# Fused local attention, spatial-gating layer and gated convolution layer on one NeuronCore: shorter input rings, an earlier split of the spatial weights and a new order of the LayerNorm steps

## The chip, the cores and the metric

The kernel runs on one core of a Trainium2 chip. The metric is the device time of one execution in microseconds (us); smaller is better.

## The reference

Three layers, one after the other, all in float32:

```python
# 1. attention, batch 2 x 8 heads, 768 positions, head size 64, in chunks of 32 queries
k_full = concat([mem_k, k[16 before the chunk : 8 after it]])     # 8 memory keys + window
a = softmax(scale * q_c @ k_full.T);  out_c = a @ v_full
# 2. spatial gating
h = gelu_tanh(x @ w_in);  u, v = h[..., :512], h[..., 512:]
v_n = (v - mean(v)) / sqrt(var(v) + 1e-6) * g_ln
v_s = einsum('ts,bsd->btd', w_sg, v_n) + b_sg
y = x + (u * v_s) @ w_out
# 3. gated convolution
h = relu(y @ w_in2);  c = 3-tap convolution of h along the sequence
result = (h * sigmoid(c)) @ w_out2
```

## The kernel before

Every engine has its own instruction list, written out in Python in the order in which it runs, and the lists are tied together by semaphores. An engine never overtakes a waiting instruction of its own.

**Products.** Each product of layers 2 and 3 is made with both operands as a high part in fp32r plus a low part (the rest), so a tile is hi·hi + hi·lo + lo·hi (`product`, L403 to L413). Weights come by DMA as 256 KB chunks into a ring of two places, `raw`. A chunk j is split by `split_hi` (L334, one copy, on ACT, POOL or DVE) and `split_lo` (L352, a subtraction, on POOL for the chunks told of here). Chunks 0 to 3 are `wv`, 4 to 7 `wu`, 8 to 16 the spatial weights `sg`, 17 on are the later layers. Chunk j may be loaded only when the low part of chunk j-2 is made (`load_chunk`, L377).

**Attention** works on 16 pairs n (two heads, half the sequence). For each pair: PE `scores(n)` (mask product and q·k); DVE `take_max`; ACT `set_bias`, eight `exps`, `guard_sum`; DVE `invert_sum`; POOL `normalise_rows` (L956, two multiplications); PE `transposes`; DVE `copy_transposed`; PE `attend`; DVE `x_parts` (L605, a cast and a subtraction that make x hi and lo); ACT `copy_x` (L768). PE runs 18 passes i (L498 to L509): in pass i it does scores of pair i, transposes of pair i-2 and attend of pair i-2 (up to pass 4 of pair i-3; pass 5 attends 2 and 3). q/k and v of a pair lie in rings of four places each; SP loads them and the chunks in one in-order list that `load_order` sorts by hand-given times (L118).

**F tiles.** From pass 6 on, PE has up to two tiles of x @ w_in in each pass (`F_SLOTS`, L73): f0 to f27, seven for each quarter of the sequence (three v tiles of 128 x 512 and four u tiles of 128 x 384; in the last quarter the u tiles f21 to f24 come first and the v tiles f25 to f27 last). The first 21 F tiles and the attend outputs share two PSUM banks in turn (`RING`), so a tile waits until the entry two before it has been evicted: f18 waits for the eviction of f17, f19 for that of f18, f20 for that of f19, f0 for `copy_x(2)`, f1 for `copy_x(3)`. ACT evicts (`evict`, L774).

**LayerNorm** has twelve v tiles i. Each goes through ACT `gelu_v(i)` (into `vw`, a ring of three 2 KB places), DVE `statistics(i)`, POOL `invert_std(i)` (an addition and a power on 128x1), DVE `normalise(i)` (L630), ACT `vn_hi_part(i)` (L803), POOL `vn_lo_part(i)` (L964). For tiles 9 to 11 the eviction is the gelu itself.

**Order around the end of attention.** Chunks 13 to 16 (`C_LATE` = 13 on) are loaded only after the last attend (`sp.wait_ge(attended, NPR)`, L390), together with the bias `b_bc`, since the `sg` weights lie where the attention's buffers were. ACT's list there (L836 to L877) mixes gelus, evictions, the four late `split_hi` and the `vn_hi_part`s. DVE's list (L649 to L667) goes statistics(i), normalise(i) one tile after the other; POOL does invert_std(i), then vn_lo_part(i). After all twelve tiles DVE turns to the gating loop (L671), which evicts the spatial products.

**Then** PE makes 16 spatial products k = 0 to 15 of 18 matmuls each (they wait for all of `sg` and for vn_lo of tiles 0 to 5, from k = 8 for all twelve; k >= 4 also waits until DVE has evicted product k-4), then the output product, and layer 3.

Of the kernel before, what the change touches and what calls it, by code (L numbers as in the profile page):

```python
# [13 lines left out]
P = 128  # L14
# [11 lines left out]
UB = 4  # L26
# [42 lines left out]
QK_RING, V_RING, A_RING, M_RING = 4, 4, 3, 4  # L69
# [45 lines left out]
POOL_HI = (1, 2, 3)  # L115


def load_order():  # L118
# [18 lines left out]
def build(nc, qk, v_win, masks, weights, g_ln, b_sg, conv_w, out):  # L137
    ctx = ExitStack()
    with ctx:
# [35 lines left out]
        qk_sb = at("qk_sb", R_B + 24 * KB, [P, QK_RING, UQ + UK], F32)  # L175
        v_sb = at("v_sb", R_B + 38 * KB, [P, V_RING, 2, UB, D], F32)
        a_sb = [at(f"a_sb{i}", R_3 + (10, 14, 28)[i] * KB, [P, 2, UB, KEYS], F32) for i in range(A_RING)]
        mask_b = at("mask_b", R_3 + 32 * KB, [P, MQ + MK], BF16)
        mask_in = at("mask_in", R_U, [P, MQ + MK], F32)
# [3 lines left out]
        vw = at("vw", R_U, [P, 3, HALF_FF], F32)  # L183
        tmp = at("tmp", R_U + 6 * KB, [P, 2, TB], F32)
# [19 lines left out]
        ends = {"attention": R_3 + 34 * KB + 512, "all": R_MISC}  # L204
# [20 lines left out]
        assert ends["attention"] <= R_RAW  # L225
# [137 lines left out]
        def _(sp):  # L363
# [38 lines left out]
        def _(pe):  # L402
# [165 lines left out]
        def _(dve):  # L568
# [47 lines left out]
            for e in range(2):  # L616
                dve.wait_ge(masks_in[e], 16)
                rows = slice(D * e, D * e + N_C)
                nc.vector.tensor_copy(mask_b[rows, :], mask_in[rows, :]).then_inc(mask_ok, 1)


            def statistics(i):
# [4 lines left out]
                link(nc.vector.bn_stats(bn6[:, i % 2, :], vw[:, i % 3, :]))  # L627
                nc.vector.bn_aggr(stats[:, i, :], bn6[:, i % 2, :]).then_inc(var_ok, 1)

            def normalise(i):  # L630
                dve.wait_ge(rstd_ok, i + 1)
                v = vw[:, i % 3, :]
                nc.vector.tensor_scalar(v, v, stats[:, i, 0:1], rstd[:, i:i + 1],  # L633
                                        ALU.subtract, ALU.mult).then_inc(vn_ok, 1)

            for i in range(NPR):
                if i == 4 or i == 5:
                    x_parts(i - 4)
                elif i > F_FROM:
                    x_parts(i - 3)  # L640
                take_max(i)
                if i >= 1:
                    invert_sum(i - 1)
                if i >= 2:
                    copy_transposed(i - 2)
                if i == 5:
                    x_parts(2)
                    x_parts(3)
            invert_sum(NPR - 1)  # L649
            statistics(0)  # L650
            x_parts(13)
            copy_transposed(14)
            normalise(0)
            statistics(1)
            normalise(1)
            statistics(2)
            x_parts(14)
            copy_transposed(15)
            normalise(2)
            statistics(3)  # L660
            normalise(3)
            statistics(4)
# [79 lines left out]
        def _(act):  # L742
# [31 lines left out]
            def evict(f):  # L774
# [15 lines left out]
            def gelu_v(i):  # L790

                act.wait_ge(free_f, TILES_R * (i // 3) + i % 3 + 1)
                if i >= 3:
                    act.wait_ge(vn_lo, i - 2)
                nc.scalar.activation(vw[:, i % 3, :], v_h[:, i, :], ACT.Gelu_apprx_tanh).then_inc(v_ok, 1)
# [7 lines left out]
            def vn_hi_part(i):  # L803
                act.wait_ge(vn_ok, i + 1)
                nc.scalar.activation(vn_r[:, 0, i, :], vw[:, i % 3, :], ACT.Copy).then_inc(vn_hi, 1)  # L805


            for e in range(2):
                act.dma_start(mask_in[D * e:D * e + N_C, :], masks).then_inc(masks_in[e], 16)
# [4 lines left out]
            for i in range(NPR):  # L814
# [6 lines left out]
                elif i == F_FROM:  # L821
                    copy_x(2)
# [3 lines left out]
                if i in SPLIT_ATTN and SPLIT_ATTN[i] not in POOL_HI:  # L826
                    split_hi(act, SPLIT_ATTN[i])
# [19 lines left out]
            split_hi(act, C_LATE)
            gelu_v(4)
            evict(19)
            vn_hi_part(3)  # L850
            gelu_v(5)
            copy_x(15)
            split_hi(act, C_LATE + 1)
            vn_hi_part(4)
            evict(20)
            gelu_v(6)
            split_hi(act, C_LATE + 2)
            vn_hi_part(5)
            gelu_v(7)
            evict(21)  # L860
            for d in range(KT):
                gelu_u(0, d)
            evict(22)
            vn_hi_part(6)
            gelu_v(8)
            split_hi(act, C_LATE + 3)
            evict(23)
            vn_hi_part(7)
            evict(24)
            vn_hi_part(8)  # L870
            for d in range(KT):
                gelu_u(1, d)
            for i in range(9, B * ST):
                evict(16 + i)
                vn_hi_part(i)
# [63 lines left out]
        def _(pool):  # L939
# [38 lines left out]
            for i in range(NPR + 1):  # L978
                if i >= 1:
                    normalise_rows(i - 1)  # L980
                if i in SPLIT_ATTN:
                    if SPLIT_ATTN[i] in POOL_HI:
                        split_hi(pool, SPLIT_ATTN[i])
                    split_lo(pool, SPLIT_ATTN[i])
# [101 lines left out]
```

## Time and profile before

| | us |
|---|---|
| median of 3 runs (lowest, highest) | 371.62 (370.39, 374.22) |
| the profiled execution | 371.19 |
| its span, first to last instruction | 369.2 |
| PE busy in the span | 342.8 (93%) |
| DVE, ACT, POOL busy | 184.7, 173.7, 129.7 |
| mean granted TensorE clock | 0.972 of 2.4 GHz |

The profiled execution is 2.0 us longer than its span; what lies around the span is taken as unchanged. The chain of waits that ended last is 71% line L410 (the products on PE). So PE is the bound on the whole, and a gain can only come from stretches in which PE waits or runs at the lower clock. Read the windows first, then PE's timeline in the stretch where its busy share falls, then the engine named behind each arrow.

### The profile page before, as it was taken

Reading aid. Unit: us, or ns where it says so; the run is one execution under the profiler, and the core shown is the slowest. Engines: PE = TensorE matmul, PEld = TensorE weight load, DVE = VectorE, ACT = ScalarE, POOL = GpSimd, SP = SyncE. Lnnn points to the kernel's source line nnn. Section 1 sums busy time; section 2 is a strip of 40 time slices with the busy share of each in tenths; the row PEclk is TensorE's granted clock in tenths of the full one; section 3 lists DMA queues with packets and bytes.
Section 4 is the critical chain, followed back from the end, with each engine's and each line's share of the span. In section 5 each row is a group of like instructions: output and inputs, shape, how many; then the busy total and the mean of one; then the engine's idle time right before and its main releaser. Section 6 shows DMA issues by size and latency. Waiting matters only on the chain.

```text
span 369.2 us, 5746 instructions
## 1 busy us (share of the span) xinstructions
PE 342.8 (93%) x2196; PEld 314.7 (85%) x2196; DVE 184.7 (50%) x273; ACT 173.7 (47%) x500; POOL 129.7 (35%) x140
## 2 busy tenths in 40 slices
PE   7678999999974696899999999999999999999997
PEld 7466798798864695899999999999999998888886
DVE  3575454453445434498544443269999995000000
ACT  2999667677652564220000222378888883011101
POOL 2597335435254465676433787500000000000000
PEclk9899999999997599899999999999999999999999
DMA  7568252351001210102000032201111001111011
GB/s 261 205 219 254 100 186 108 107 166 33 2 0 51 78 29 28 28 31 58 30 0 2 28 83 61 57 30 28 51 37 28 2 0 45 43 58 57 30 57 57
DMA packets 12279, 25.18 MB, mean 68 GB/s; under 512 B 1622, under 2 KB 1878, under 8 KB 12252
## 3 DMA queue, kind: packets, MB, share of 16 engines
q1 hardware_dynamic: 12240, 24.79, 20.3%
q8 instruction: 17, 0.28, 0.3%
q14 instruction: 10, 0.08, 0.1%
q10 hardware_dynamic: 12, 0.03, 0.0%
HBM read 21.67 MB, written 3.15 MB: 67 GB/s over the span
## 4 chain that ended last, share of the span: by engine, by line
PE 78%; POOL 8%; issue 4%; ACT 4%; DVE 3%; DMA 2%; SPq 0%; POOLq 0%; ACTq 0%
PE psum L410 71%; DMA raw<-weights 2%; PE psum L492 2%; PE psum L466 2%; POOL vn_r L968 2%; DVE vw L633 2%; PE psum L480 2%; POOL a_sb L961 1%; ACT vn_r L805 1%; POOL wv_r L358 1%; POOL rstd L974 1%; PE psum L461 1%; ACT a_sb L757 1%; POOL wu_r L358 1%; ACT u_x L800 0%
## 5 line engine op out<-in xcount | busy, mean ns | idle before, releaser
L410 PE MATMUL psum<-y_r,i_hi 128*128 128x384 f32 x256 | 64.9, 334 | 0.0
L410 PE MATMUL psum<-sg_r,vn_r 128*128 128x384 f32 x288 | 51.7, 341 | 5.0 <-POOL sg_r L358 5.0
L410 PEld LDWEIGHTS psum<-sg_r,vn_r 128*128 128x128 f32 x288 | 51.4, 193 | 5.4 <-POOL sg_r L358 5.4
L410 PE MATMUL psum<-x_r,wu_r 128*128 128x384 f32 x192 | 40.6, 368 | 9.8 <-ACT u_x L787 9.8
L961 POOL TENSOR_TENSOR a_sb<-a_sb,rinv 96x512 f32<-96x512 f32 x32 | 32.6, 1037 | 48.2 <-DVE rinv L596 48.2
L410 PEld LDWEIGHTS psum<-x_r,wu_r 128*128 128x128 f32 x192 | 37.0, 209 | 11.0 <-ACT u_x L787 10.4
L410 PEld LDWEIGHTS psum<-y_r,i_hi 128*128 128x128 f32 x256 | 46.1, 188 | 0.0
L757 ACT ACTIVATE a_sb<-psum,bias 96x128 f32<-96x128 f32 x128 | 44.8, 363 | 0.5
L410 PE MATMUL psum<-y_r,i_lo 128*128 128x384 f32 x128 | 42.8, 334 | 0.0
L883 ACT ACTIVATE y_r<-yw 128x384 fp32r<-128x384 f32 x16 | 8.4, 526 | 67.9 <-DVE yw L698 67.9
L410 PE MATMUL psum<-wv_r,x_r 128*128 128x512 f32 x144 | 35.5, 398 | 1.4 <-POOL wu_r L358 1.4
L410 PE MATMUL psum<-gated_r,wo_r 128*128 128x384 f32 x192 | 33.4, 334 | 0.0
L410 PEld LDWEIGHTS psum<-gated_r,wo_r 128*128 128x128 f32 x192 | 33.3, 188 | 0.0
L410 PEld LDWEIGHTS psum<-wv_r,x_r 128*128 128x128 f32 x144 | 26.3, 188 | 7.2 <-POOL wu_r L358 1.5
L934 ACT ACTIVATE ob<-psum 128x512 f32<-128x512 f32 (+1 forms) x13 | 7.3, 564 | 49.4 <-PE psum L410 49.4
L410 PE MATMUL psum<-o_hi,hg_r 128*128 128x512 f32 x96 | 29.7, 389 | 0.0
L757 ACT ACTIVATION_READ_ACCUMULATOR a_sb<-psum,bias 96x1 f32 x128 | 25.9, 202 | 0.0
L994 POOL TENSOR_TENSOR gated_r<-u_x,gated_r 128x384 fp32r<-128x384 f32 x16 | 16.6, 1040 | 22.4 <-DVE gated_r L686 22.4
L410 PEld LDWEIGHTS psum<-y_r,i_lo 128*128 128x128 f32 x128 | 24.0, 188 | 0.0
L603 DVE COPY at_sb<-psum 128x768 f32<-128x768 f32 x16 | 15.1, 943 | 17.7 <-PE psum L480 17.5
L968 POOL TENSOR_TENSOR vn_r<-vw,vn_r 128x512 fp32r<-128x512 f32 x12 | 15.6, 1301 | 20.1 <-ACT vn_r L805 20.1
L587 DVE TENSOR_REDUCE negmax<-psum 96x8 f32<-96x1024 f32 x16 | 19.5, 1220 | 6.0 <-PE psum L466 5.2
(86 smaller groups left out, 581.5 us busy)
## 6 DMA issues: line engine op xcount, KB each, us to landing
raw<-weights SPq DMA_DIRECT2D x37, 256.0 KB, 2.7
qk_sb<-qk SPq DMA_DIRECT2D x16, 448.0 KB, 4.7
v_sb<-v_win SPq DMA_DIRECT2D x16, 256.0 KB, 4.3
result<-ob SPq DMA_DIRECT2D x11, 256.0 KB, 2.0
b_bc<-b_sg SPq DMA_DIRECT2D x1, 384.0 KB, 4.0
result<-ob SPq DMA_DIRECT2D x2, 128.0 KB, 1.7
mask_in<-masks ACTq DMA_DIRECT2D x2, 13.1 KB
g_sb<-g_ln SPq DMA_DIRECT2D x1, 2.0 KB, 2.7
```

The source lines that it names most:

```text
L358: eng.tensor_tensor(chunk_dst(j, 1), raw[:, j % 2, :], f32(chunk_dst(j, 0)), ALU.subtract).then_inc(w_lo, 1)
L410: last = nc.tensor.matmul(psum[0:m, bank, 0:n], stat(a, t), mov(b, t), start=(t == 0 and i == 0), stop=(t == tiles - 1 and i == 2))
L466: last = nc.tensor.matmul(psum[0:QB, bank + e, j * KEYS:(j + 1) * KEYS], qk_sb[rows, s, j * QB:(j + 1) * QB], qk_sb[rows, s, UQ + j * KEYS ...
L480: last = nc.tensor.transpose(psum[:, 4 + e, j * QB:(j + 1) * QB], a_sb[n % A_RING][0:QB, e, j, :], ident[0:QB, :])
L492: last = nc.tensor.matmul(psum[D * e:D * e + D, o_bank(n), j * QB:(j + 1) * QB], v_sb[:, s, e, j, :], at_sb[:, n % 2, e, j * QB:(j + 1) * QB],
L587: nc.vector.tensor_reduce(out=negmax[0:QB, n % M_RING, :], in_=psum[0:QB, bank:bank + 2, :].rearrange("p s (j k) -> p (s j) k", j=UB), axi ...
L603: nc.vector.tensor_copy(at_sb[:, n % 2, :, :], psum[:, 4:6, 0:UQ]).then_inc(at_copied, 1)
L757: nc.scalar.activation(a_sb[n % A_RING][0:QB, e, j, :], psum[0:QB, 2 * (n % 2) + e, j * KEYS:(j + 1) * KEYS], ACT.Exp, bias=bias[0:QB, n % ...
L883: nc.scalar.activation(y_r[:, b, 0, m, t0:t0 + TB], yw[:, k % 6, :], ACT.Copy)\
L961: nc.gpsimd.tensor_tensor(a, a, r.broadcast_to([QB, UB, KEYS]), ALU.mult)\
L968: nc.gpsimd.tensor_tensor(vn_r[:, 1, i, :], vw[:, i % 3, :], f32(vn_r[:, 0, i, :]), ALU.subtract).then_inc(vn_lo, 1)
L994: nc.gpsimd.tensor_tensor(gated_at(r, 1, d), u_at(r, d), f32(gated_at(r, 0, d)), ALU.subtract).then_inc(gated_lo, 1)
```

## The change

- The rings of q/k and v shrink from 4 to 3 places. The attention's buffers and the mask move out of the place of the `sg` weights; `vw` grows to 4 places, and two of the three `a_sb` buffers now lie under it. So gelu_v(0) waits for the transposes of pair 13 and gelu_v(2) for those of pair 14.
- All spatial chunks, 8 to 16, are split during attention: ACT does split_hi(j) in pass j (16 behind the last pass), POOL split_lo(j) behind normalise_rows(j-1). Nothing of them waits for the last attend any more.
- Chunks 1 and 2 are split on POOL before normalise_rows(0), chunk 3 before normalise_rows(1); they were behind pairs 0, 1 and 2.
- SP's list is new: the second half of the mask first, then chunks and q/k, v in another order. The mask is converted in two pieces per half, and scores(0) waits for the first pieces only.
- On DVE, x_parts(0) to (3) move: in passes 4 and 5 they stand elsewhere, and take_max(5) now stands behind x_parts(3). On ACT copy_x(2) goes from pass 6 to pass 5.
- LayerNorm: DVE does statistics(i) and then normalise(i-1); POOL invert_std(i+1) before vn_lo_part(i). ACT's evictions come earlier against the gelus.

The core of the diff:

```diff
-QK_RING, V_RING, A_RING, M_RING = 4, 4, 3, 4
+QK_RING, V_RING, A_RING, M_RING = 3, 3, 3, 4
...
-EARLY_SG = 5
-C_LATE = C_SG + EARLY_SG
-SPLIT_ATTN = {1: 1, 2: 2, 3: 3, 4: 4, 5: 5, 6: 6, 7: 7, 9: 8, 10: 9, 11: 10, 12: 11, 13: 12}
+SPLIT_BEFORE = {1: 0, 2: 0, 3: 1}
+SPLIT_AFTER = {4: 4, 5: 5, ... 15: 15, 16: 16}
...
+    first = [("qk", 0), ("chunk", 0), ("qk", 1), ("chunk", 1), ("qk", 2), ("chunk", 2), ("v", 0),
+             ("qk", 3), ("chunk", 3), ("v", 1), ("qk", 4), ("v", 2), ("chunk", 4), ("qk", 5), ("v", 3)]
+    attended_at = {n: i for i in range(ATTN_STEPS) for n in attends(i)}
     for p in range(NPR):
-        events.append((p - 10.2 if p < QK_RING else p - QK_RING + 0.5, ("qk", p)))
-        events.append((p - 8.9 if p < V_RING else p - V_RING + 3.5, ("v", p)))
+        events.append((p - QK_RING + 0.2, ("qk", p)))
+        events.append((attended_at[p - V_RING] + 0.9 if p >= V_RING else 0, ("v", p)))
...
-        vw = at("vw", R_U, [P, 3, HALF_FF], F32)
+        vw = at("vw", R_U, [P, 4, HALF_FF], F32)
...
-            if C_LATE <= j < C_O:
-                eng.wait_ge(transposed, 2 * NPR)
-            elif C_O <= j < C_I2:
+            if C_O <= j < C_I2:
...
+            sp.dma_start(mask_in[D:D + N_C, :], masks).then_inc(masks_in[1], 16)
...
-            for j in range(C_LATE, N_CHUNK):
-                if j == C_LATE:
+            for j in range(C_O, N_CHUNK):
+                if j == C_O:
                     sp.wait_ge(attended, NPR)
...
             for i in range(NPR):                      # DVE
...
+                if i == 5:
+                    x_parts(1)
+                    copy_transposed(3)
+                    invert_sum(4)
+                    x_parts(2)
+                    x_parts(3)
+                    take_max(5)
+                    continue
...
-            normalise(4)
-            for i in range(5, B * ST):
+            for i in range(2, B * ST):
                 statistics(i)
-                normalise(i)
+                normalise(i - 1)
+            normalise(B * ST - 1)
...
             def gelu_v(i):
-                if i >= 3:
-                    act.wait_ge(vn_lo, i - 2)
+                if i >= 4:
+                    act.wait_ge(vn_lo, i - 3)
+                elif i == 0:
+                    act.wait_ge(transposed, 2 * (NPR - 2))
+                elif i == 2:
+                    act.wait_ge(transposed, 2 * (NPR - 1))
...
+            invert_std(0)                             # POOL
             for i in range(B * ST):
-                invert_std(i)
-                if i in (4, 6, 8, 9):
-                    split_lo(pool, C_LATE + (4, 6, 8, 9).index(i))
+                if i + 1 < B * ST:
+                    invert_std(i + 1)
                 vn_lo_part(i)
```

PE's instruction list is the same before and after. Three places where the lists of the others differ:

ACT behind the last exps, before. `v_h` is the copied v tile, `vw<-v_h` a gelu, `u_x<-psum` the eviction of a u tile, `x_f` copy_x, `vn_r` the high part of a LayerNorm tile, `sg_r<-raw` a split_hi:

```order
L795 ACTIVATE vw<-v_h 128x512
L805 ACTIVATE vn_r<-vw 128x512
L787 ACTIVATE u_x<-psum 128x384
L771 ACTIVATE x_f<-psum 128x384
L795 ACTIVATE vw<-v_h 128x512
L805 ACTIVATE vn_r<-vw 128x512
L347 ACTIVATE sg_r<-raw 128x512
L795 ACTIVATE vw<-v_h 128x512
L787 ACTIVATE u_x<-psum 128x384
L805 ACTIVATE vn_r<-vw 128x512
```

The same stretch after:

```order
L791 ACTIVATE u_x<-psum 128x384
L803 ACTIVATE vw<-v_h 128x512
L775 ACTIVATE x_f<-psum 128x384
L803 ACTIVATE vw<-v_h 128x512
L348 ACTIVATE sg_r<-raw 128x512
L791 ACTIVATE u_x<-psum 128x384
L803 ACTIVATE vw<-v_h 128x512
L775 ACTIVATE x_f<-psum 128x384
L813 ACTIVATE vn_r<-vw 128x512
L803 ACTIVATE vw<-v_h 128x512
L791 ACTIVATE u_x<-psum 128x384
```

In the piece before, the first eviction is f18 and the second f19, with a split_hi between them. After, the three evictions are f17, f18 and f19, and the only split_hi left, that of chunk 16, stands ahead of the eviction of f18.

POOL at the start, before (`a_sb` is normalise_rows, `wv_r<-raw` a high part, `wv_r<-raw,wv_r` a low part):

```order
L358 TENSOR_TENSOR wv_r<-raw,wv_r 128x512
L961 TENSOR_TENSOR a_sb_62<-a_sb_62,rinv 96x512 x2
L349 CAST wv_r<-raw 128x512
L358 TENSOR_TENSOR wv_r<-raw,wv_r 128x512
L961 TENSOR_TENSOR a_sb_63<-a_sb_63,rinv 96x512 x2
L349 CAST wv_r<-raw 128x512
L358 TENSOR_TENSOR wv_r<-raw,wv_r 128x512
```

And after:

```order
L359 TENSOR_TENSOR wv_r<-raw,wv_r 128x512
L350 CAST wv_r<-raw 128x512
L359 TENSOR_TENSOR wv_r<-raw,wv_r 128x512
L350 CAST wv_r<-raw 128x512
L359 TENSOR_TENSOR wv_r<-raw,wv_r 128x512
L969 TENSOR_TENSOR a_sb_62<-a_sb_62,rinv 96x512 x2
L350 CAST wv_r<-raw 128x512
L359 TENSOR_TENSOR wv_r<-raw,wv_r 128x512
L969 TENSOR_TENSOR a_sb_63<-a_sb_63,rinv 96x512 x2
```

Two chunks are now split ahead of the first pair's normalise_rows, and the third ahead of the second pair's.

DVE in pass 5, before (`negmax` is take_max, `rinv` invert_sum, `at_sb` copy_transposed, a CAST and a TENSOR_TENSOR on `x_r` one x_parts):

```order
L608 CAST x_r<-psum 128x384
L611 TENSOR_TENSOR x_r<-psum,x_r 128x384
L587 TENSOR_REDUCE negmax<-psum 96x8
L596 RECIPROCAL rinv<-rowsum_e 96x8
L603 COPY at_sb<-psum 128x768
L608 CAST x_r<-psum 128x384
L611 TENSOR_TENSOR x_r<-psum,x_r 128x384
L608 CAST x_r<-psum 128x384
L611 TENSOR_TENSOR x_r<-psum,x_r 128x384
```

And after:

```order
L610 CAST x_r<-psum 128x384
L613 TENSOR_TENSOR x_r<-psum,x_r 128x384
L605 COPY at_sb<-psum 128x768
L598 RECIPROCAL rinv<-rowsum_e 96x8
L610 CAST x_r<-psum 128x384
L613 TENSOR_TENSOR x_r<-psum,x_r 128x384
L610 CAST x_r<-psum 128x384
L613 TENSOR_TENSOR x_r<-psum,x_r 128x384
L589 TENSOR_REDUCE negmax<-psum 96x8 x2
```

The maximum of pair 5 went from ahead of three x_parts' worth of work to behind it, next to the maximum of pair 6.

## Rows read from the trace of the kernel before

**Rows 1.** Windows: stretch, its length, busy us by engine, PEclk, DMA share, GB/s.

```profile
108.00:117.00 9.00, 5.42 (x39) 4.79 (x36) 4.87 (x11) 3.39 (x7) 5.63 (x8) 0.81 0.00 0
117.00:126.00 9.00, 2.98 (x9) 2.99 (x10) 2.59 (x6) 3.58 (x7) 2.84 (x5) 0.59 0.31 102
...
180.00:369.00 189.00, 186.66 (x1011) 176.10 (x1009) 90.21 (x125) 73.39 (x118) 34.29 (x32) 1.00 0.12 37
```

**Rows 2.** Timeline of PE, 93 to 152: start, length, instruction, [idle before <-releaser].

```profile
104.69 2.38 PE L410 MATMUL psum<-x_r,wu_r 128*128 128x384 f32 x12 [0.23 <-ACT u_x L787]
107.20 0.88 PE L492 MATMUL psum<-at_sb,v_sb 128*64 128x96 f32 x16
...
112.21 3.72 PE L410 MATMUL psum<-x_r,wu_r 128*128 128x384 f32 x12 [3.31 <-ACT u_x L787]
...
123.02 13.35 PE L410 MATMUL psum<-x_r,wu_r 128*128 128x384 f32 x60 [6.28 <-ACT u_x L787]
...
149.51 2.93 PE L410 MATMUL psum<-sg_r,vn_r 128*128 128x384 f32 x8 [4.95 <-POOL sg_r L358]
```

**Rows 3.** Timeline of ACT, same stretch.

```profile
111.68 0.47 ACT L787 ACTIVATE u_x<-psum 128x384 f32<-128x384 f32 x1
...
113.38 0.62 ACT L795 ACTIVATE vw<-v_h 128x512 f32<-128x512 f32 x1
114.70 0.63 ACT L805 ACTIVATE vn_r<-vw 128x512 fp32r<-128x512 f32 x1 [0.69 <-DVE vw L633]
121.44 0.63 ACT L347 ACTIVATE sg_r<-raw 128x512 fp32r<-128x512 f32 x1 [6.11 <-DMA raw<-weights]
...
122.49 0.47 ACT L787 ACTIVATE u_x<-psum 128x384 f32<-128x384 f32 x1
```

**Rows 4.** Timeline of SP's queue, 0 to 152: the load of chunks 13 and on.

```profile
117.15 32.67 SPq L381 DMA_DIRECT2D raw<-weights  x6
```

**Rows 5.** Chain of waits in order of time: a u tile of 12 matmuls.

```profile
49.01 2.14 PE psum L410 x12
```

**Rows 6.** Timeline of DVE, 93 to 152.

```profile
111.85 0.52 DVE L608 CAST x_r<-psum 128x384 fp32r<-128x384 f32 x1
...
112.88 0.95 DVE L603 COPY at_sb<-psum 128x768 f32<-128x768 f32 x1
114.12 0.55 DVE L633 TENSOR_SCALAR vw<-vw,stats,rstd 128x512 f32<-128x512 f32 x1 [0.29 <-POOL rstd L974]
...
125.83 1.49 DVE L633 TENSOR_SCALAR vw<-vw,stats,rstd 128x512 f32<-128x512 f32 x1 [1.26 <-POOL rstd L974]
127.24 0.68 DVE L627 BATCH_NORM_STATS2 bn<-vw 128x6 f32<-128x512 f32 x1
127.96 0.18 DVE L628 BATCH_NORM_AGGREGATE stats<-bn 128x2 f32<-128x6 f32 x1
```

**Rows 7.** Timeline of POOL, 80 to 152: a split_lo, a vn_lo_part and the invert_std behind it.

```profile
125.76 1.28 POOL L358 TENSOR_TENSOR sg_r<-raw,sg_r 128x512 fp32r<-128x512 f32 x1
128.06 1.28 POOL L968 TENSOR_TENSOR vn_r<-vw,vn_r 128x512 fp32r<-128x512 f32 x1 [1.02 <-ACT vn_r L805]
...
129.73 0.57 POOL L974 TENSOR_TENSOR rstd<-var_e,half_neg 128x1 f32<-128x1 f32 x1
```

**Rows 8.** Timeline of DVE, 140 to 200: eviction of a spatial product.

```profile
176.26 0.62 DVE L678 SCALAR_TENSOR_TENSOR tmp<-psum,g_sb,b_bc 128x384 f32<-128x384 f32 x1 [1.18 <-PE psum L410]
```

**Rows 9.** Timeline of all engines, 0 to 50: the start, and the first F tiles.

```profile
4.72 0.73 DVE L619 CAST mask_b<-mask_in 3x1120 bf16<-3x1120 f32 x1 [0.66 <-DMA mask_in<-masks]
...
28.33 0.36 ACT L757 ACTIVATE a_sb<-psum,bias 96x128 f32<-96x128 f32 x1
...
29.99 0.56 DVE L611 TENSOR_TENSOR x_r<-psum,x_r 128x384 fp32r<-128x384 f32 x1
...
31.93 3.02 PE L410 MATMUL psum<-wv_r,x_r 128*128 128x512 f32 x12 [1.35 <-POOL wu_r L358]
...
35.39 3.01 PE L410 MATMUL psum<-wv_r,x_r 128*128 128x512 f32 x12
```

More of the change, by code:

```diff
@@ L201, in build @@
         ob = at("ob", R_RAW, [P, 2, DM], F32)
-        ends = {"attention": R_3 + 34 * KB + 512, "all": R_MISC}
+        ends = {"attention": R_VL + 22 * KB + 768, "all": R_MISC}
         def small(name, shape, used_by="all"):
@@ L224, in build @@
         rinv = small("rinv", [P, M_RING, 2 * UB], "attention")
-        assert ends["attention"] <= R_RAW
+        assert ends["attention"] <= R_D
         bn6 = small("bn6", [P, 2, 6])
@@ L618, in _ @@
                 rows = slice(D * e, D * e + N_C)
-                nc.vector.tensor_copy(mask_b[rows, :], mask_in[rows, :]).then_inc(mask_ok, 1)
+                nc.vector.tensor_copy(mask_b[rows, 0:MQ + UK], mask_in[rows, 0:MQ + UK]).then_inc(mask_ok, 1)
+            for e in range(2):
+                rows = slice(D * e, D * e + N_C)
+                nc.vector.tensor_copy(mask_b[rows, MQ + UK:], mask_in[rows, MQ + UK:]).then_inc(mask_ok, 1)
             def statistics(i):
@@ L643, in _ @@
                     invert_sum(i - 1)
+                if i == 4:
+                    x_parts(0)
                 if i >= 2:
                     copy_transposed(i - 2)
-                if i == 5:
-                    x_parts(2)
-                    x_parts(3)
             invert_sum(NPR - 1)
-            statistics(0)
             x_parts(13)
             copy_transposed(14)
+            statistics(0)
+            x_parts(14)
+            copy_transposed(15)
             normalise(0)
             statistics(1)
[L655 to L662, printed above, removed]
             x_parts(15)
-            normalise(4)
-            for i in range(5, B * ST):
+            for i in range(2, B * ST):
                 statistics(i)
-                normalise(i)
+                normalise(i - 1)
+            normalise(B * ST - 1)
             dve.wait_ge(vectors_in, 48)
@@ L804, in vn_hi_part @@
                 act.wait_ge(vn_ok, i + 1)
-                nc.scalar.activation(vn_r[:, 0, i, :], vw[:, i % 3, :], ACT.Copy).then_inc(vn_hi, 1)
-            for e in range(2):
-                act.dma_start(mask_in[D * e:D * e + N_C, :], masks).then_inc(masks_in[e], 16)
+                nc.scalar.activation(vn_r[:, 0, i, :], vw[:, i % 4, :], ACT.Copy).then_inc(vn_hi, 1)
+            act.dma_start(mask_in[0:N_C, :], masks).then_inc(masks_in[0], 16)
             act.wait_ge(half_ok, 1)
@@ L821, in _ @@
                 elif i == F_FROM:
-                    copy_x(2)
                     copy_x(3)
@@ L825, in _ @@
                     copy_x(i - 3)
-                if i in SPLIT_ATTN and SPLIT_ATTN[i] not in POOL_HI:
-                    split_hi(act, SPLIT_ATTN[i])
+                if i == 5:
+                    copy_x(2)
+                for j in SPLIT_AFTER:
+                    if SPLIT_AFTER[j] == i:
+                        split_hi(act, j)
                 set_bias(i)
@@ L833, in _ @@
                 guard_sum(i)
+            evict(17)
             gelu_v(0)
-            evict(17)
             copy_x(13)
             gelu_v(1)
+            split_hi(act, 16)
+            evict(18)
+            gelu_v(2)
+            copy_x(14)
             vn_hi_part(0)
-            gelu_v(2)
+            gelu_v(3)
+            evict(19)
             vn_hi_part(1)
-            evict(18)
-            copy_x(14)
-            gelu_v(3)
+            copy_x(15)
+            gelu_v(4)
+            evict(20)
             vn_hi_part(2)
-            split_hi(act, C_LATE)
-            gelu_v(4)
-            evict(19)
+            gelu_v(5)
+            evict(21)
             vn_hi_part(3)
-            gelu_v(5)
-            copy_x(15)
-            split_hi(act, C_LATE + 1)
+            gelu_u(0, 0)
+            gelu_u(0, 1)
             vn_hi_part(4)
-            evict(20)
+            evict(22)
+            gelu_u(0, 2)
+            gelu_u(0, 3)
             gelu_v(6)
-            split_hi(act, C_LATE + 2)
             vn_hi_part(5)
+            evict(23)
             gelu_v(7)
[L860 to L863, printed above, removed]
             vn_hi_part(6)
             gelu_v(8)
-            split_hi(act, C_LATE + 3)
-            evict(23)
+            evict(24)
             vn_hi_part(7)
-            evict(24)
-            vn_hi_part(8)
             for d in range(KT):
@@ L977, in _ @@
             split_lo(pool, 0)
[L978 to L984, printed above, removed]
+            for i in range(NPR):
+                for j in SPLIT_BEFORE:
+                    if SPLIT_BEFORE[j] == i:
+                        split_hi(pool, j)
+                        split_lo(pool, j)
+                normalise_rows(i)
+                for j in SPLIT_AFTER:
+                    if SPLIT_AFTER[j] == i + 1:
+                        split_lo(pool, j)
+            invert_std(0)
             for i in range(B * ST):
-                invert_std(i)
-                if i in (4, 6, 8, 9):
-                    split_lo(pool, C_LATE + (4, 6, 8, 9).index(i))
+                if i + 1 < B * ST:
+                    invert_std(i + 1)
                 vn_lo_part(i)
```

47 lines of the change are left out of this document (24 added, 23 removed).

## The prediction

> **What bounds the kernel now.** I read the windows first. From 180 on PE is busy for 186.66 of 189 us at the full granted clock (1.00, its 2.4 GHz level), but in 108 to 117 it is busy for 5.42 of 9 and in 117 to 126 for 2.98 of 9, with the granted clock at 0.81 and 0.59 on average [rows 1]. So I look for PE's idle time there. PE's timeline names it: f19 starts at 112.21 behind 3.31 us of idle, f20 at 123.02 behind 6.28 us, the first spatial product at 149.51 behind 4.95 us [rows 2]. The clock fell too: f19's twelve matmuls took 3.72 us, f18's 2.38 [rows 2], while 2.14 is what such a tile takes in the chain of waits [rows 5].
>
> Why f20 waits is in ACT's list. It needs the eviction of f19 (122.49), and that stood behind the split_hi of chunk 13, which sat 6.11 us until its DMA had landed at 121.44 [rows 3]. The load was issued at 117.15 only, after the last attend [rows 4]. f19 waited for an eviction (111.68) behind the high part of LayerNorm tile 1. The 4.95 us before the first spatial product end with the low part of chunk 16, the last of four late splits.
>
> **The change, part by part.** I keep the clock of the profiled run and walk the new lists through it.
>
> *1. From the last exps to f20.* PE's list is the same; what changes is when evictions come. The eviction of f17 now stands ahead of the gelus, so f18 starts at about 104.4 instead of 104.69 and ends 2.38 later, at 106.7. Behind it ACT evicts f18 (by 107.2) and PE does attend(14) (0.88 [rows 2]), to 107.5. Then the chain is, in row durations: DVE x_parts(14), 0.52 [rows 6] and 0.56 [rows 9], to 108.65; copy_transposed(15), 0.95, to 109.6; normalise(0), 0.55 [rows 6], to 110.15; ACT the high part of tile 0, 0.63, to 110.8; gelu_v(3), 0.62, of which 0.1 overlaps, to 111.3; eviction of f19, 0.47, to 111.7 [rows 3]. PE meanwhile has the transposes, f19 and attend(15), until 111.3. So f20 starts at 111.7 in place of 123.02: 11.3 us gained. Split_hi(16) stands ahead of the eviction of f18, but its chunk waits only for attend(12) and split_lo(14), done by about 96; with the 4.3 us that the late load took (117.15 to 121.44 [rows 3, 4]) it lands by 101 and is asked for at 106. The added POOL step, split_lo(16), 1.28 [rows 7], ends at 108.0, and invert_std(0) at 109.0, still 0.6 before normalise(0). The new waits of gelu_v(0) and (2) for transposes cost nothing: those of pair 13 end near 100.6, of pair 14 near 104.5.
>
> *2. f20 to f27.* The sixty matmuls of f20 to f24 took 13.35 [rows 2], part of it at the lower clock. PE now idles only 0.4 us before them, so I take 5 x 2.14 = 10.7 [rows 5]: 2.65 gained. If the clock is low all the same, this gain is nil. f25 to f27 took 149.51 - 4.95 - 136.4 = 8.2 to 8.4 [rows 2], the same after. End: 111.7 + 10.7 + 8.35 = 130.75.
>
> *3. The spatial weights.* split_lo(16) ends at 108, long before 130.75. The 4.95 us go. Two further waits could take their place. (a) vn_lo of tiles 0 to 5: POOL's new order gives one tile every 0.96 (invert_std with its gaps, 129.34 to 130.30 [rows 7]) + 1.28 + 0.1 = 2.3 us from 112.0 on. Tile 5 is later, since its statistics partner gelu_v(6) stands behind eight other ACT steps: gelu_v(6) at 122.6, low part of tile 5 at 126.7, 4 us before it is needed. (b) DVE starts evicting spatial products only after normalise(11), and the fifth product (k = 4) needs the first evicted. A round from gelu_v(i) to gelu_v(i+1) is gelu 0.62 + statistics 0.68 + 0.18 + normalise 0.55 [rows 6] + high part 0.63, in all 2.7 us; with an eviction in the first, the four u gelus (each like a u eviction, 0.47 [rows 3] less some overlap, 1.75) in the third and the wait for rstd in the last, six rounds are 3.05 + 2.7 + 4.3 + 2.65 + 2.65 + 3.1 = 18.45. From 122.6 that is 141.0; with the first eviction (0.62 [rows 8]) 141.6. A spatial product is 18/12 of a u tile, 3.2 us, so k = 4 wants to start at 130.75 + 12.8 = 143.6. Margin 2 us: no wait.
>
> Start of the spatial products: 149.51 to 130.75, **18.75 us gained**. Everything behind is PE at its full clock in an unchanged order, 186.66 of 189 us busy [rows 1], and stays.
>
> *4. The start.* Both mask halves come on their own queue and only the first pieces are converted before scores(0): the second cast, 4.72 to 5.45 [rows 9], could end about 1.3 us earlier if q/k is there too. But it reaches the F tiles only through POOL and ACT. POOL still has one chunk (0.6 + 1.28) between pairs 0 and 1, so normalise_rows(1) is hardly earlier. x_parts(0) now waits for invert_sum(3), so ACT's copy_x(0) and exps(4) come about 0.6 us later. And in pass 5 DVE takes the maximum of pair 5 only after x_parts(3), whose subtraction ran until 30.55 [rows 9]: maximum to about 31.6, exps(5) from 31.85 instead of 28.33, copy_x(3) at 35.0 to 35.45. PE: f0, no longer behind copy_x(2) of pass 6 (the releaser that the row names, a POOL split, was done earlier), starts at 30.5 instead of 31.93, but f1 needs copy_x(3): 35.5 against 35.39 [rows 9]. What f0 gains is idle time before f1. Best case 1.3 us gained; worst case PE, idle before f0, runs f0 at the lower clock and with what follows loses 2.6 (twice 3.72 - 2.38 [rows 2]). I take 0.4 lost, near the walk's 0.1.
>
> *5. Rings of three and the added splits.* Nine passes carry a split_hi more or other than before. ACT had idle time ahead of nearly every set_bias, and PE is gapless from 31.93 on; cost nil. A pass is (104.69 - 31.93)/10 = 7.3 us [rows 2, 9]. q/k of pair p is now asked for three passes ahead instead of four, v when the pair three before is attended, two passes and more ahead of its use: each above the 4.3 us of a load. I cost this at nil, with a rival below.
>
> **Sum.** 371.19 - 18.75 + 0.4 = 352.85 for an execution like the profiled one. The median of the runs is 0.43 above the profiled execution, so 353.3.
>
> **A rule of the skill against the change.** The trace shows normalise at 0.55 us alone and at 1.49 when it started 0.07 us behind a POOL split of 1.28 [rows 6, 7]; it ended 0.28 behind POOL's end. In the old order POOL's vn_lo_part(i) followed normalise(i) and could not meet it. In the new one POOL turns to vn_lo_part right when rstd is out and normalise may start. The Trainium skill says why, in "SBUF — State Buffer", section "Who interferes with whom": DVE's two-port modes, in which a tensor_scalar can run, and GpSimd hold one port pair for a whole instruction, and whoever comes second waits. By that rule the trace's 1.49 agrees.
>
> **Rivals.**
> *A, the LayerNorm ends too late (0.18).* Each collision costs normalise 1.49 - 0.55 = 0.94. For tiles 2 to 4 I walked with them (they are within the 122.6). If all six rounds behind meet POOL too, 6 x 0.94 = 5.6, less 2 of margin: k = 4 waits 3.6 us, and the next twelve matmuls may run as f19 did, 1.3 more. Time 353.3 + 4.9 = 358. For it: both engines are set free by the same statistics. Against it: in these rounds POOL's low part comes behind the high part, during the next gelu, and only the short power (0.57 [rows 7]) can meet normalise.
> *B, the start is worse (0.12).* The 2.6 us of step 4: 355.5. For it: exps(5) is 3.5 us late, and there is a new PE gap of about 2 us before scores(6) and one before f1. Against: PE's passes from 7 on have no ACT-bound step.
> *C, loads come late (0.04), slower than before.* SP's list is in order: chunk j stands behind v(j-1), which waits for the attend at the end of pass j-2, and ACT wants chunk j in pass j ahead of the exps of pair j. The slack is about a pass less the load, 7.3 - 4.3 = 3 us. If loads took more than 7.3 us, each of the nine passes 7 to 15 would wait; at 3 us each 27 us are lost against 18.75 gained: 380. It turns slower from 2.1 us a pass. Against: the old list used the same order for chunks 8 to 12, and PE shows no gap.
> *D, the gain is smaller because the clock stays low behind the attention or f20 still waits for something (0.06).* Step 2's 2.65 and half of the 11.3 gone: 361.6.
>
> **Numbers.** The forecast (351 to 355) has 0.6. A measurement of this kernel tells about 1% from no change. C is the only case that is slower (0.03 by over 1%, 0.02 within 1%); all others are at least 2% faster, 0.95. The range 350.5 to 358.5 leaves out the upper part of A, C and D.
>
> **What would show it.** Right: no PE gap over 1 us between f17 and the end, clock 1.0 from 99 on, f20 within 9 us of f18's start (it was 18.3), first spatial product about 19 us earlier, no ACT wait for `raw` behind the last pass, f1 within 1 us of 35.4. Wrong: a gap before the fifth spatial product with normalise at 1.5 in the late rounds (A); f1 later than 37 (B); SP releases ahead of split_hi or scores in passes 7 to 15 (C).

## The result, and the profile after

| | before | after |
|---|---|---|
| median of 4 runs, us (lowest, highest) | 371.35 (370.39, 374.22) | 351.54 (350.50, 351.73) |
| profiled execution, its span | 371.19, 369.2 | 351.44, 349.4 |
| mean granted TensorE clock | 0.972 | 0.985 |

The ratio is 0.9438, with a 95% interval of 0.939 to 0.9486. The forecast was 353.3 with a range from 350.5: the direction and nearly all of the size were right, but 371.35 x 0.9438 is 350.48, just under the lower edge of the range. The kernel gained more than forecast. How much more depends on the measure: the ratio of the two medians is 0.9467, the two profiled executions differ by 19.8 us where the forecast had 18.35, and the changed kernel timed again later gave 0.949 and 0.9466. So the size of the miss is read from the two profiles below.

PE's timeline of the changed kernel from f16 (98.05) to the output product, to be held against [rows 2] (start, length, instruction, idle before it and who ended it; left out are transposes and f17):

```profile
98.05 3.02 PE L412 MATMUL psum<-wv_r,x_r 128*128 128x512 f32 x12
...
105.24 2.36 PE L412 MATMUL psum<-x_r,wu_r 128*128 128x384 f32 x12
107.53 0.88 PE L494 MATMUL psum<-at_sb,v_sb 128*64 128x96 f32 x16
...
109.00 2.36 PE L412 MATMUL psum<-x_r,wu_r 128*128 128x384 f32 x12
111.29 0.88 PE L494 MATMUL psum<-at_sb,v_sb 128*64 128x96 f32 x16
112.54 10.70 PE L412 MATMUL psum<-x_r,wu_r 128*128 128x384 f32 x60 [0.37 <-ACT u_x L791]
123.08 8.36 PE L412 MATMUL psum<-wv_r,x_r 128*128 128x512 f32 x36
131.28 50.11 PE L412 MATMUL psum<-sg_r,vn_r 128*128 128x384 f32 x288
181.22 19.05 PE L412 MATMUL psum<-gated_r,wo_r 128*128 128x384 f32 x109
```

The three waits of [rows 2], 3.31, 6.28 and 4.95 us, are gone; 0.37 is left ahead of f20. The windows of the same stretch, against [rows 1] (length, busy us of PE, PEld, DVE, ACT, POOL, granted clock, DMA share, GB/s):

```profile
108.00:117.00 9.00, 8.63 (x71) 8.08 (x68) 7.89 (x15) 4.61 (x11) 6.46 (x10) 1.00 0.37 104
117.00:126.00 9.00, 9.00 (x49) 8.49 (x49) 5.81 (x9) 5.95 (x13) 7.09 (x11) 1.00 0.00 0
```

But for the 0.37 us PE is busy throughout, at the 2.4 GHz level. The start is the one place that became worse. PE's timeline after, to be held against the last group of rows ahead of the prediction, [rows 9]:

```profile
14.34 1.81 PE L482 MATMUL psum<-ident,a_sb 96*128 96x96 f32 x8 [2.00 <-POOL a_sb L969]
...
29.32 0.93 PE L494 MATMUL psum<-at_sb,v_sb 128*64 128x96 f32 x16 [2.20 <-ACT x_f L775]
30.19 0.66 PE L463 MATMUL psum<-mask_b 64*96 64x512 bf16 x2
30.64 1.91 PE L468 MATMUL psum<-qk_sb 64*96 64x128 f32 x16
32.49 3.44 PE L412 MATMUL psum<-wv_r,x_r 128*128 128x512 f32 x12
35.76 0.82 PE L482 MATMUL psum<-ident,a_sb 96*128 96x96 f32 x8
36.41 3.00 PE L412 MATMUL psum<-wv_r,x_r 128*128 128x512 f32 x12
```

f1 starts at 36.41, 1.02 us later than before (35.39). From the two profiles the 19.8 us of span come out as follows:

| stretch | before | after | gained | forecast |
|---|---|---|---|---|
| start to f1 | 35.39 | 36.41 | -1.02 | -0.4 |
| f1 to f20 | 87.63 | 76.13 | 11.50 | 11.3 |
| f20 to the first spatial product | 26.49 | 18.74 | 7.75 | 7.4 |
| from there to the end | 219.7 | 218.1 | 1.6 | 0 |

The four gains add up to 19.8 and the forecasts to 18.3. The last line is what the forecast lacked. Before, the 288 matmuls of the spatial products took 51.66 us, after 50.11. That is 1.55 of the 1.6. The granted clock in the windows of before, from 149.5 on and then from 158.5 on:

```profile
149.50:158.50 9.00, 8.98 (x43) 8.99 (x44) 4.50 (x10) 3.68 (x8) 4.88 (x7) 0.82 0.12 30
158.50:167.50 9.00, 9.00 (x54) 9.00 (x53) 8.79 (x13) 0.84 (x3) 7.22 (x7) 1.00 0.09 31
```

PE had idled 4.95 us there and then did 43 matmuls in the first window and 54 in the second, at the same busy share.

### The profile page after: what moved, and what is told of

Read it like the earlier page. It is cut to its first block, busy times and chain, and to the rows that moved or that the text cites. A ratio compares the mean times of both kernels' runs of the same rounds, so it can differ in the third digit from the quotient of the medians.

```text
span 349.4 us, 5751 instructions
## 1 busy us (share of the span) xinstructions
PE 337.5 (97%) x2196; PEld 310.0 (89%) x2196; DVE 186.9 (54%) x275; ACT 173.5 (50%) x500; POOL 132.4 (38%) x140
## 4 chain that ended last, share of the span: by engine, by line
PE 92%; ACT 2%; POOL 2%; DMA 1%; DVE 1%; issue 1%; SPq 0%; POOLq 0%; ACTq 0%
PE psum L412 81%; PE psum L468 3%; PE psum L482 3%; PE psum L494 3%; DMA raw<-weights 1%; PE psum L463 1%; POOL wv_r L359 1%; ACT a_sb L761 1%; POOL wv_r L350 0%; DVE negmax L589 0%; POOL a_sb L969 0%; DVE x_r L610 0%; DVE at_sb L605 0%; ACT wv_r L348 0%; ACT vn_r L813 0%
## 5 line engine op out<-in xcount | busy, mean ns | idle before, releaser
L412 PE MATMUL psum<-sg_r,vn_r 128*128 128x384 f32 x288 | 50.1, 334 | 0.0
L412 PEld LDWEIGHTS psum<-sg_r,vn_r 128*128 128x128 f32 x288 | 50.0, 188 | 0.1
L412 PE MATMUL psum<-x_r,wu_r 128*128 128x384 f32 x192 | 36.6, 342 | 0.4 <-ACT u_x L791 0.4
L412 PEld LDWEIGHTS psum<-x_r,wu_r 128*128 128x128 f32 x192 | 33.0, 188 | 1.1 <-ACT u_x L791 0.6
L412 PEld LDWEIGHTS psum<-o_hi,hg_r 128*128 128x128 f32 x96 | 18.0, 188 | 3.8
```

The lines of the kernel that those rows point to most:

```text
L412: last = nc.tensor.matmul(psum[0:m, bank, 0:n], stat(a, t), mov(b, t), start=(t == 0 and i == 0), stop=(t == tiles - 1 and i == 2))
```

## The experiments

Four runs ask where the 19.8 us came from, and seven what the start costs. The time of before on the same chips was 371.66 (first four), 371.41 (a0, c1, c2, c3) and 371.54 (the last three).

**The late load of the spatial weights alone.** In the changed kernel, with the loop of SP behind the last attend, the split_hi on ACT and the split_lo on POOL:

```diff
-SPLIT_AFTER = {4: 4, ... 12: 12, 13: 13, 14: 14, 15: 15, 16: 16}
+SPLIT_AFTER = {4: 4, ... 12: 12}
+C_LATE = C_SG + 5
...
-            for j in range(C_O, N_CHUNK):
+            for j in range(C_LATE, N_CHUNK):
...
             vn_hi_part(0)
+            split_hi(act, C_LATE)
             gelu_v(3)
             evict(19)
             vn_hi_part(1)
             copy_x(15)
+            split_hi(act, C_LATE + 1)
...
+                if i in (3, 4, 6, 8):
+                    split_lo(pool, C_LATE + (3, 4, 6, 8).index(i))
                 vn_lo_part(i)
```

> The changed kernel with chunks 13 to 16 of the spatial weights loaded after the last attend and split behind the LayerNorm tiles, as before; all else as changed. Theory (the late load stalled ACT's in-order list and with it the evictions): the load is issued near 112.5, lands 4.3 us later near 117, the eviction of f19 comes near 118 instead of 112.0, so f20 starts 5 to 6 us later and its first matmuls run at the lower clock (1 to 2.5 us more); the last low part comes after f27, so the spatial products wait some us more. In all 8 to 14 us slower than the changed kernel: 360 to 366. Rival (the LayerNorm order and the four vw places bring the gain, the late load was only the last of several waits): at most 2 us slower, 353 to 354.

Measured: 366.84 us, 15 slower than the changed kernel, just above the range expected; ratio to before 0.987 (0.9843 to 0.9896). Its PE timeline:

```profile
119.57 12.79 PE L413 MATMUL psum<-x_r,wu_r 128*128 128x384 f32 x60 [6.19 <-ACT u_x L792]
132.20 8.36 PE L413 MATMUL psum<-wv_r,x_r 128*128 128x512 f32 x36
146.27 52.59 PE L413 MATMUL psum<-sg_r,vn_r 128*128 128x384 f32 x288 [5.71 <-POOL sg_r L360]
```

Both waits of before are back, with the eviction and the spatial split as their releasers. f1 was at 37.60 in this run, 1.2 later than in the profile of the changed kernel; less that, f20 is 5.8 us late (112.54 + 1.2 against 119.57). The sixty matmuls take 2.1 more, the wait for the split 5.7, the products at the lower clock 2.5. The theory of the first wait stands: ACT's list stood 5.19 us until the load had landed at 117.99, and the LayerNorm order cannot save the kernel from that. The second wait is less simple. The high part of chunk 16 was done at 138.3, but its low part came at 144.95 only, behind LayerNorm steps in POOL's list. So those 5.71 us come from where this run puts the late splits, and the run, which moves load and splits together, does not tell the two apart.

**The LayerNorm order alone.**

```diff
             x_parts(15)
+            normalise(1)
             for i in range(2, B * ST):
                 statistics(i)
-                normalise(i - 1)
-            normalise(B * ST - 1)
+                normalise(i)
...
-            invert_std(0)
             for i in range(B * ST):
-                if i + 1 < B * ST:
-                    invert_std(i + 1)
+                invert_std(i)
                 vn_lo_part(i)
```

> The changed kernel with LayerNorm in the order of before on DVE (statistics(i), normalise(i)) and POOL (invert_std(i), vn_lo_part(i)); loads, splits and ACT's list as changed. Theory of the walk (a serial tile costs 3.6 us, an interleaved one 2.3 to 2.7, and the fifth spatial product needs DVE free by about 144): low part of tile 5 comes near 131 to 134, so the spatial products start 0 to 3 us later, and the fifth waits until DVE is through, near 152: 5 to 10 us slower than the changed kernel, 357 to 361. Rival (LayerNorm had slack, its order is worth nothing): 351.5.

Measured, in two executions: 362.31 us, 10.8 slower than the changed kernel and above the 357 to 361 expected; ratio to before 0.975 (0.9676 to 0.9824). PE's timeline:

```profile
134.74 12.67 PE L412 MATMUL psum<-sg_r,vn_r 128*128 128x384 f32 x72
152.86 40.46 PE L412 MATMUL psum<-sg_r,vn_r 128*128 128x384 f32 x216 [5.46 <-DVE tmp L682]
```

After exactly 72 matmuls, four products, PE waits 5.46 us for DVE's first eviction: the fifth product, as the forecast's walk had it. The other 216 matmuls take 40.46 where 216/288 of 50.11 would be 37.6: the lower clock again. In this profile f1 stood at 38.41, so 2.0 us of its length are the start, which the edit does not touch. The interval of the ratio does not meet that of the changed kernel: the LayerNorm order was necessary too. The two parts are not to be added (15 and 11 us are more than 19.8): each bounds the same stretch once the other is mended.

**Idle time and clock.** One wait moved in the changed kernel:

```diff
-                pe.wait_ge(vn_lo, ST * (b + 1))
+                pe.wait_ge(vn_lo, 9 if r < 2 else 12)
```

> The changed kernel, but the first spatial product waits for the low parts of nine LayerNorm tiles instead of six, near 137 instead of 131.3: 5.8 us of idle on PE and nothing else. Theory (the idle time also lowers the granted clock for the first products behind it, which the forecast left out): 7.0 to 8.0 us slower than the changed kernel, the extra 1.2 to 2.2 us seen as a granted clock under 1 in the 9 us behind the wait and in a longer time for the 288 matmuls. Rival (only the idle time itself): 5.8 us slower.

Measured, in two executions: 360.91 us, 9.4 slower; ratio to before 0.9712 (0.9614 to 0.981). The products behind the wait, and the windows from 135 on:

```profile
139.34 53.00 PE L412 MATMUL psum<-sg_r,vn_r 128*128 128x384 f32 x288 [5.68 <-issue]
```

```profile
135.00:144.00 9.00, 4.66 (x15) 4.69 (x16) 4.87 (x10) 3.72 (x7) 6.58 (x10) 0.71 0.00 0
144.00:153.00 9.00, 9.00 (x49) 9.00 (x48) 5.78 (x10) 2.29 (x5) 4.98 (x5) 0.91 0.13 32
```

53.00 against 50.11: 2.9 us on top of the 5.68 idle, more than the 1.2 to 2.2 expected, and the granted clock was 0.71 and 0.91 in the two windows. The profiled execution is 11.0 us longer than that of the changed kernel: 8.8 of it lie between f20 and the end, 2.2 in its start (f1 at 38.62), which the edit does not touch. The rival, 5.8 us and nothing else, falls. And the counterpart, in the kernel before, takes no wait away and only keeps PE at work while it waits:

```diff
+            pe.wait_ge(at_copied, NPR)
+            pe.wait_ge(x_full, NPR)
+            pe.wait_ge(free_f, F_LAST)
+            for _ in range(2):
+                product(7, P, TB, lambda h, t: wu_r[:, h, t, 0:P],
+                        lambda h, t: x_r[:, h, t, 3 * TB:4 * TB], KT)
             for r in range(2 * B):
```

> The kernel before, with 24 more matmuls (two tiles, result unused) in PE's idle time ahead of the first spatial product, which lasted 4.95 us; they take 4.3 us. No wait goes. Theory (about 1.6 us of what the change gained behind the start of the spatial products is clock alone): 1.3 to 2 us faster than before, granted clock 1.00 in 144 to 162 instead of 0.81 in the first half. Rival: no faster than before, or slower by the part of the matmuls that does not fit, 0 to 0.5 us.

Measured: 370.32 us against 371.66, ratio 0.9955 (0.9919 to 0.999): 1.3 us faster by 24 matmuls more.

```profile
143.93 4.35 PE L410 MATMUL psum<-x_r,wu_r 128*128 128x384 f32 x24
149.02 50.22 PE L410 MATMUL psum<-sg_r,vn_r 128*128 128x384 f32 x288 [0.74 <-POOL sg_r L358]
```

The products take 50.22, as in the changed kernel (50.11) and not as before (51.66), and the granted clock from 144 on is 1.00, not 0.81:

```profile
144.00:153.00 9.00, 8.26 (x48) 7.94 (x47) 3.79 (x6) 3.02 (x8) 5.16 (x7) 1.00 0.16 58
```

Since the 288 matmuls and their list are those of before, the 1.55 us behind the start of the spatial products are clock. The medians of the spans differ by more than those of the times, 367.4 against 369.7: this run has 2.1 to 3.6 us outside its span where before has 2.0. Why is open.

**The start.** The changed kernel again, as a yardstick on the same chip:

> The changed kernel itself, timed beside the three variants of its start on one chip: 351.5, as measured.

Measured 352.13 (ratio 0.949, 0.9445 to 0.9535), f1 at 37.57. The next three runs have four executions each and were timed beside this one. First the split of chunks 2 and 3 each one pair later:

```diff
-SPLIT_BEFORE = {1: 0, 2: 0, 3: 1}
+SPLIT_BEFORE = {1: 0, 2: 1, 3: 2}
```

> The changed kernel with chunk 2 split behind normalise_rows(0) and chunk 3 behind normalise_rows(1) (only chunk 1 stays ahead of the first pair). Theory (in the changed kernel normalise_rows(0) waits on POOL for chunk 2 from 11.4 to 13.2, the transposes of pair 0 behind it on PE hold scores(3), and exps(3) starts 2 us late): f1 starts near 34.4 instead of 36.4, 1.5 to 2.2 us faster than the changed kernel. Rival (the start is set by what follows, x_parts(0) and take_max(5)): within 0.4 us of the changed kernel.

Measured 348.96 us, ratio to before 0.9422 (0.9386 to 0.9459): 3.2 us under the changed kernel beside it, more than the 1.5 to 2.2 expected, and the two intervals just overlap. Its PE timeline:

```profile
12.16 0.52 PE L482 MATMUL psum<-ident,a_sb 96*128 96x96 f32 x4 [0.39 <-POOL a_sb L969]
...
28.77 3.02 PE L412 MATMUL psum<-wv_r,x_r 128*128 128x512 f32 x12
31.63 0.82 PE L482 MATMUL psum<-ident,a_sb 96*128 96x96 f32 x8
33.75 3.02 PE L412 MATMUL psum<-wv_r,x_r 128*128 128x512 f32 x12 [1.30 <-ACT x_f L775]
```

The transposes of pair 0 start at 12.16, not 14.34, and f1 at 33.75, not 36.41. Now f1 waits 1.30 us for copy_x(3), as the walk of the prediction had said. The other part of the start, on DVE and, in the last lines, on ACT:

```diff
-                if i == 5:
-                    x_parts(1)
-                    copy_transposed(3)
-                    invert_sum(4)
-                    x_parts(2)
-                    x_parts(3)
-                    take_max(5)
-                    continue
+                if i == 4 or i == 5:
+                    x_parts(i - 4)
...
                 if i >= 2:
                     copy_transposed(i - 2)
+                if i == 5:
+                    x_parts(2)
+                    x_parts(3)
...
                 elif i == F_FROM:
+                    copy_x(2)
                     copy_x(3)
-                if i == 5:
-                    copy_x(2)
```

> The changed kernel with x_parts(0) to (3), take_max(5) and copy_x(2) in the places of before. Theory of the walk (take_max(5) behind x_parts(3) delays exps(5) by 3 us, but f1 then only needs copy_x(3), so little is won while exps(3) is late): 0.3 to 1.0 us faster than the changed kernel, exps(5) near 28.8 instead of 32.8. Rival (the new places help, since f0 starts earlier by them): 0.5 to 1.5 us slower.

Measured 349.68 us (0.943, 0.9399 to 0.9462), 2.4 us under the changed kernel beside it, more than the 0.3 to 1.0 expected; here too the intervals just overlap. f1 at 34.90. In the changed kernel PE idles 2.20 us ahead of attend(3), and in all three profiles of it the matmuls behind are slow (30.64 with 1.91 above, against 1.04 in this run at 29.06). That part of the gain was not in the walk. Both together:

> Both reverts of the start, c1 and c2, in the changed kernel, with the early mask kept. Theory: ACT's exps run without a gap to pair 5, f0 starts near 30 and f1 near 33.4: 2.5 to 3.3 us faster than the changed kernel, 348.3 to 349. Rival (a load of the shorter rings or a split of wu takes the place of the wait): at most 1.5 us faster.

Measured 349.26 us (0.9413, 0.9377 to 0.9448), 2.9 under the changed kernel. f1 at 32.75 came 0.7 before the time expected, and the span of the profiled execution, 345.8, is the shortest of all profiled ones; but the median is no better than that of c1 alone. What c1 and c2 give does not add up (3.2 and 2.4 against 2.9). In a second set with more rounds:

> The changed kernel again, as the yardstick of the next two on this chip: 351 to 352.5.

> c3_both again with more rounds, to give the 2 to 3 us between it and the changed kernel an interval: 348.5 to 349.5. Rival (the difference was noise): within 0.5 us of the changed kernel.

> c3_both with copy_x(2) moved in ACT's list to between the two halves of the exps of pair 5 (x_lo of pair 2 is ready at 26.8, the first half ends near 27.1). Theory (what is left before f0 is only that f0 waits 1.34 us for copy_x(2) behind the second half): f0 starts near 27.9 instead of 29.3, f1 near 31.4 instead of 32.75, all 1.0 to 1.4 us faster than c3. Rival (ACT or the split of wu then holds f1 or f3, so that it is given back): 0 to 0.4 us.

The edit of the last one, against c3:

```diff
                 elif i == F_FROM:
-                    copy_x(2)
                     copy_x(3)
...
                 if f1 is not None:
                     evict(f1)
+                if i == 5:
+                    copy_x(2)
                 exps(i, 1)
```

| same chip, us | median | ratio to before | f0, f1 |
|---|---|---|---|
| changed kernel | 351.09 | 0.9466 (0.9436 to 0.9496) | 31.65, 35.57 |
| c3 again | 348.49 | 0.9388 (0.936 to 0.9416) | 30.17, 33.62 |
| c4 | 347.56 | 0.9361 (0.9335 to 0.9388) | 29.43, 32.93 |

c3 and the changed kernel have intervals that do not meet. c4 is 0.9 us under c3, a little less than expected, and their intervals overlap. Its profile shows the mechanism: f0 follows scores(6) with no wait, where c3 waited 1.36 us.

```profile
27.39 0.88 PE L494 MATMUL psum<-at_sb,v_sb 128*64 128x96 f32 x16 [1.49 <-DVE at_sb L605]
...
29.43 3.06 PE L412 MATMUL psum<-wv_r,x_r 128*128 128x512 f32 x12
32.93 3.01 PE L412 MATMUL psum<-wv_r,x_r 128*128 128x512 f32 x12
```

From attend(3) to f0 it needs 2.04 us, c3 3.46 (26.71 to 30.17), which is the expected 1.4; the start up to there was 0.7 later in this execution. c4 beats both kernels: 347.56 against 371.54 and 351.09.

## Why the prediction came out as it did

The forecast had 18.35 us of gain and the profiles show 19.8. The difference is 1.6 behind the start of the spatial products, 0.3 and 0.2 between f1 and there, less 0.6 that the start lost beyond the forecast. That the start hid part of the error is luck.

**Step 1, to f20 (11.3): right.** Measured 11.5 between f1 and f20. ACT's list after, between the last exps and f20, in the order of the chain:

```profile
107.64 0.49 ACT L791 ACTIVATE u_x<-psum 128x384 f32<-128x384 f32 x1
108.03 0.62 ACT L803 ACTIVATE vw<-v_h 128x512 f32<-128x512 f32 x1
109.64 0.49 ACT L775 ACTIVATE x_f<-psum 128x384 f32<-128x384 f32 x1 [1.00 <-DVE x_r L613]
110.96 0.63 ACT L813 ACTIVATE vn_r<-vw 128x512 fp32r<-128x512 f32 x1 [0.82 <-DVE vw L638]
111.50 0.61 ACT L803 ACTIVATE vw<-v_h 128x512 f32<-128x512 f32 x1
112.02 0.47 ACT L791 ACTIVATE u_x<-psum 128x384 f32<-128x384 f32 x1
```

Less the 1.0 us by which everything stands later, the high part of tile 0 is at 109.96 and the eviction of f19 ends at 111.5; forecast 110.15 and 111.7. That the late load was the root of this wait is shown by e1.

**Step 2, f20 to f27: right.** 10.70 for the sixty matmuls, forecast 10.7; 8.2 for the rest.

**Step 3, the spatial weights: its first half right, its last sentence wrong.** Both waits that could have taken the place stayed away, but with less room than forecast. DVE's first eviction started at 142.30, against a forecast 141.0 + 1.0 for the late start, and four products of 50.11/16 from 131.28 on end at 143.8: room 0.9 us with the eviction's 0.60, not 2. One collision, that of tile 11 (below), took 1.0 of it. e2 shows how real this wait is. The sentence "Everything behind is PE at its full clock in an unchanged order, 186.66 of 189 us busy [rows 1], and stays" is the step that failed. It put this term at nothing, and it measured 1.6: it read the clock from the window 180 to 369 alone, and the products began at 149.51. The idle time in front of them had a second price, 1.55 us, as part of the products ran at the 1.2 GHz level (0.82 granted in the 9 us behind it), and taking the idle time away gave that back too. e5 shows this alone (50.22 us for the products with every wait of before left in but this one filled), e4 shows it with the sign reversed (53.00). The forecast had used the same reading for f20 (step 2) and not here.

**Step 4, the start (0.4 lost): direction right, mechanism half right.** Measured 1.0 lost in the first profile, 2.2 and 0.2 in the other two. The early mask gave 1.0 us (scores(0) at 4.50 against 5.51), and exps(5) came late, at 32.85 where the walk had 31.85; f0, walked to 30.5, came at 32.49. Two things were missed. POOL could not start normalise_rows(0) before 13.16, since chunk 2 came late and its split stood ahead; the transposes of pair 0 wait for it on PE ahead of scores(3) (2.00 us above), and ACT idled 2.01 us ahead of the bias of pair 3. The forecast's step looked only at the split between pairs 0 and 1. Second, PE's idle 2.20 us ahead of attend(3) put scores(6) and f0 at the lower clock (1.91 and 3.44 against 1.04 and 3.02), which I kept as rival B. Taking both parts back gave 2.6 us with intervals that do not meet (c3 again); c1 and c2, at 3.2 and 2.4, point the same way but do not settle what each part alone costs.

**Step 5, rings and splits: right.** PE has no gap from f0 to f19 in the first profile of the changed kernel, and no load is a releaser in passes 7 to 15.

**The rivals.** A did not happen, but not for lack of collisions; the rule on which it rests holds. DVE's normalise after:

```profile
114.11 0.52 DVE L638 TENSOR_SCALAR vw<-vw,stats,rstd 128x512 f32<-128x512 f32 x1
...
115.39 1.55 DVE L638 TENSOR_SCALAR vw<-vw,stats,rstd 128x512 f32<-128x512 f32 x1
...
124.82 0.52 DVE L638 TENSOR_SCALAR vw<-vw,stats,rstd 128x512 f32<-128x512 f32 x1
...
140.84 1.54 DVE L638 TENSOR_SCALAR vw<-vw,stats,rstd 128x512 f32<-128x512 f32 x1 [0.77 <-POOL rstd L982]
```

Tiles 2, 3 and 4 took 1.54 to 1.55, as walked; those at 115.39 and 140.84 each began beside a vn_lo_part (next fence). Tiles 5 to 10 took 0.52. Tile 11, costed at 0.55, took 1.54, half of the room that the walk had. B is what the first and the second profile of the changed kernel show in part. C and D fell: no load is late from pass 7 on, and the clock was 1.00 from 36 on.

## What to carry to other kernels

When a wait in front of a long run of matmuls goes, price the matmuls behind it too: look at the granted clock in the window that begins where the wait ends, not in a window far behind. When work is moved forward into the idle time of an engine, find the first instruction behind it in the list, and ask who in another in-order list is queued behind that one; here a 1.9 us split ahead of a 2 us step cost a bound engine 2 us. Two parts of a change that bound the same stretch must both be there, and a test that undoes each alone shows more than the whole.

## What was not expected of the hardware

**Who comes first matters, also for small instructions.** POOL's timeline after, the additions of invert_std and two vn_lo_parts:

```profile
111.83 0.21 POOL L981 TENSOR_SCALAR var_e<-stats 128x1 f32<-128x1 f32 x1 [1.79 <-DVE stats L633]
...
115.36 1.29 POOL L976 TENSOR_TENSOR vn_r<-vw,vn_r 128x512 fp32r<-128x512 f32 x1
...
124.99 0.42 POOL L981 TENSOR_SCALAR var_e<-stats 128x1 f32<-128x1 f32 x1 [1.39 <-DVE stats L633]
...
140.81 1.29 POOL L976 TENSOR_TENSOR vn_r<-vw,vn_r 128x512 fp32r<-128x512 f32 x1
```

Where DVE's normalise started just ahead (124.82), it kept its 0.52 and POOL's 128x1 addition took 0.42 in place of 0.21. Where POOL's subtraction was 0.03 us ahead (115.36 against 115.39, 140.81 against 140.84), normalise waited and took 1.5. The Trainium skill has this in "SBUF — State Buffer", section "Who interferes with whom": issue order decides who blocks. The rows agree, and show it for an instruction of one element per partition.

**The price of the lower clock is not fixed.** Behind 4.95 us of idle the products lost 1.55 us, behind 5.46 (e2) and 5.68 (e4) 2.9, behind 5.71 (e1) 2.5. What sets the size within this is open.

**The start scatters.** f1 of the changed kernel as it stands was at 36.41, 37.57 and 35.57 in three profiles, with a granted clock of 0.72, 0.52 and 0.69 in the window 9 to 18. In that window c1 and c3 had 1.00 in their first profiles, c3 again 0.82, c2 0.69 and c4 0.62. The idle time in the window does not order them: c4 waits there once, for 2.02 us, and c1 3.7 us in six pieces. Over whole executions the kernels do differ: the mean granted clock was 0.976 to 0.985 in all 14 of the changed kernel and 0.985 to 1.00 in the 23 of c1 to c4, so clock goes along with what these variants gain. Which execution falls to the lower level was not settled, and no run was made for it alone.
